# Last mean summed on TensorE, two reciprocals moved from items 1 and 2 to items 5 and 6, x in twelve chunks

## The reference, cut to what matters

```python
x = fft2(x).real                      # x: (2, 3008, 256), over sequence and feature axes
x = x.reshape(6016, 256)
rms = sqrt(mean(x * x, -1) + 1e-6);  xn = x / rms * rms_g
g = xn @ w_gate;  v = xn @ w_val      # 256 -> 1536
x = (g * sigmoid(g) * v) @ w_out      # 1536 -> 256
h = x @ w_in                          # 256 -> 2048
out = (h * cos(h)) @ w_out2           # 2048 -> 256
```

## Time and profile before

| | us |
|---|---|
| median of 3 runs | 985.58 |
| the profiled execution | 985.71 |
| its span in the trace | 983.6 |
| TensorE (PE) busy | 972.8 (99%) |
| VectorE (DVE) busy | 743.0 |
| ScalarE (ACT) busy | 640.0 |
| GpSimd (POOL) busy | 350.5 |

### The profile page before, as it was taken

One profiled execution on the slowest core, in us unless ns is written; L12 is line 12 of the kernel. 1 busy time (PEld: TensorE's weight loads), 2 busy tenths in 40 slices (PEclk: granted clock), 3 DMA queues, 4 the chain that ended last, 5 costly groups with the idle time before them and its releaser, 6 DMA issues.

```text
span 983.6 us, 13016 instructions
## 1 busy us (share of the span) xinstructions
PE 972.8 (99%) x4518; PEld 808.3 (82%) x4518; DVE 743.0 (76%) x1031; ACT 640.0 (65%) x805; POOL 350.5 (36%) x292
## 2 busy tenths in 40 slices
PE   8999999999999999999999999999999999999998
PEld 7987878888888888888888888888888888888886
DVE  6889877768876768877768887667887767887665
ACT  5586778765368774458775448775448776437777
POOL 0378864027730007750007751005661004770000
PEclk9999999999999999999999999999999999999999
DMA  9889001001010001010001010001000000000001
GB/s 326 241 209 246 1 5 50 0 1 43 1 43 1 1 0 42 1 36 6 0 1 42 0 32 11 0 0 42 0 32 0 0 0 3 39 0 0 0 0 42
DMA packets 14082, 36.80 MB, mean 37 GB/s; under 512 B 2618, under 2 KB 6682, under 8 KB 13658
## 3 DMA queue, kind: packets, MB, share of 16 engines
q1 hardware_dynamic: 11978, 31.63, 9.6%
q0 software_dynamic: 2064, 4.72, 2.6%
HBM read 22.35 MB, written 9.26 MB: 32 GB/s over the span
## 4 chain that ended last, share of the span: by engine, by line
PE 95%; DVE 3%; DMA 1%; ACT 1%; SPq 0%; issue 0%; DVEq 0%
PE ps L546 31%; PE ps L548 30%; PE ps L547 30%; PE ps L497 2%; DMA x_sb<-x 1%; PE ps L515 1%; PE ps L513 1%; DVE h_lo L1002 0%; DVE plus L1017 0%; SPq L323 0%; DVE x_sb L907 0%; DVE work L1025 0%; PE ps L482 0%; DVE work L1026 0%; DVE h_lo L1010 0%; PE ps L531 0%
## 5 line engine op out<-in xcount | busy, mean ns | idle before, releaser
L546 PE MATMUL ps<-h_hi,wo_hi 128*128 128x502 f32 x672 | 261.7, 389 | 0.6 <-DVE h_lo L1002 0.5
L548 PE MATMUL ps<-h_hi,wo_lo 128*128 128x502 f32 x672 | 261.6, 389 | 0.0
L547 PE MATMUL ps<-h_lo,wo_hi 128*128 128x502 f32 x672 | 261.0, 388 | 0.0
L1116 POOL TENSOR_TENSOR h_lo<-work,h_hi 128x502 fp32r<-128x502 f32 x92 | 102.7, 1124 | 374.7 <-ACT h_hi L800 373.2
L785 ACT ACTIVATE h_hi<-work 128x502 fp32r<-128x502 f32 x132 | 82.3, 626 | 174.3 <-POOL work L1205 174.2
L1103 DVE SCALAR_TENSOR_TENSOR work<-work,ps 128x1004 f32<-128x1004 f32 (+1 forms) x109 | 117.1, 1075 | 97.5 <-ACT work L885 96.9
L1087 DVE SCALAR_TENSOR_TENSOR work<-work,ps 128x1004 f32<-128x1004 f32 (+1 forms) x109 | 116.5, 1074 | 48.0 <-ACT work L871 48.0
L546 PE MATMUL ps<-x_hi,win_hi 128*128 128x502 f32 x384 | 150.1, 391 | 1.3 <-DVE work L1103 1.3
L547 PE MATMUL ps<-x_lo,win_hi 128*128 128x502 f32 x384 | 149.4, 389 | 0.0
L546 PEld LDWEIGHTS ps<-h_hi,wo_hi 128*128 128x128 f32 x672 | 126.3, 188 | 28.1 <-DVE h_lo L1002 1.1
L548 PE MATMUL ps<-x_hi,win_lo 128*128 128x502 f32 x384 | 149.1, 388 | 0.0
(11 more groups left out here) (90 smaller groups left out, 1279.2 us busy)
## 6 DMA issues: line engine op xcount, KB each, us to landing
out<-y_sb SPq DMA_DIRECT2D x10, 502.0 KB, 3.1
x_sb<-x SPq DMA_DIRECT2D x6, 768.0 KB, 10.9
w_lo<-w_f POOLq DMA_DIRECT2D x6, 512.0 KB, 7.8
uv_t<-uv_dram SPq DMA_DIRECT2D x6, 502.0 KB, 3.7
wo_raw<-wo SPq DMA_DIRECT2D x1, 2048.0 KB, 8.8
win_raw<-win SPq DMA_DIRECT2D x1, 2048.0 KB, 9.1
raw_b<-w1b SPq DMA_DIRECT2D x3, 512.0 KB, 12.6
raw_a<-w1a SPq DMA_DIRECT2D x3, 512.0 KB, 12.9
```

The lines of the kernel that those rows point to most:

```text
L546: nc.tensor.matmul(acc, w_hi, v_hi, start=start, stop=False)
L547: nc.tensor.matmul(acc, w_hi, v_lo, start=False, stop=False)
L548: return nc.tensor.matmul(acc, w_lo, v_hi, start=False, stop=stop)
L1116: nc.gpsimd.tensor_tensor(dst, src, hi.bitcast(F32), ALU.subtract).then_inc(s, 1)
```

## The change

x comes in twelve chunks, and the nine columns m that are folded by half lie elsewhere (chunks 3, 5 and 8 with 3 columns each; before: chunks 3 and 5 with 3 each and chunk 10 with 1). The rows of the second batch's four parts are 5, 4, 4, 4 in place of 4, 4, 4, 5. The ninth mean no longer waits for an addition on GpSimd: TensorE accumulates the product of plane 1 and that of plane 0, and its place is after item 3 in place of item 4 of tile 0. The reciprocals of groups 1 and 2 stand in items 5 and 6 of the second network in place of 1 and 2.

```diff
-CHUNKS = [1, 1, 1, 3, 3, 3, 3, 3, 3, 2, 1]
-HALF_FOLDED = (3, 5, 10)
+CHUNKS = [1, 1, 1, 3, 2, 3, 1, 3, 3, 2, 3, 1]
+HALF_FOLDED = (3, 5, 8)
-PARTS = [[3, 3, 4, 4, 3], [4, 4, 4, 5]]
+PARTS = [[3, 3, 4, 4, 3], [5, 4, 4, 4]]
-        LAST_MEAN_AT = 4
+        LAST_MEAN_AT = 3
@@ rms(q), TensorE
-                pe.wait_ge(sq_added, q + 1)
+                if q < MEANS - 1:
+                    pe.wait_ge(sq_added, q + 1)
+                else:
+                    pe.wait_ge(sq_done, q + 1)
...
-                    nc.tensor.matmul(ps[at:at + QUARTER, rms_bank(q), r * N2:(r + 1) * N2], mean_w,
-                                     squares[:, q % SQUARES, 0, i * N2:(i + 1) * N2], start=True, stop=True
+                    acc, cols = ps[at:at + QUARTER, rms_bank(q), r * N2:(r + 1) * N2], slice(i * N2, (i + 1) * N2)
+                    if q == MEANS - 1:
+                        nc.tensor.matmul(acc, mean_w, squares[:, q % SQUARES, 1, cols], start=True, stop=False)
+                    nc.tensor.matmul(acc, mean_w, squares[:, q % SQUARES, 0, cols], start=q < MEANS - 1, stop=True
                                      ).then_inc(ms_done, 1)
@@ tile(), VectorE, second network
-                    if first and j in (1, 2):
-                        recip(j)
+                    if first and j in (5, 6):
+                        recip(j - 4)
@@ tile(), GpSimd, first network
-                    if first and i == LAST_MEAN_AT - 1:
-                        add_squares(MEANS - 1)
```

## The result

The changed kernel takes 992.2 us (median of 5 runs, 991.4 to 992.49) against 985.58: ratio 1.0066, 95% interval 1.0051 to 1.0081. It is slower by 6.6 us. Its profiled execution takes 992.09 us with a span of 990.0, 6.38 more than that of before.

A forecast was written before the change was run, and what follows sets the result against it. TensorE, busy 972.8 of 983.6 us, was taken as the bound. From 985.71 us, gains of 1.5, 0.2 and 0.1 and a stall of 5.5 gave 989.4; the 8-in-10 range was 987.8 to 992.4.

The forecast's parts named there:

- first rival: TensorE, after the stall: the clock falls to 1.2 GHz, 2.5 us more, 991.9; chance 0.27.
- The stall: TensorE before item 8's up products: late reciprocals delay `scale_uv`, then ScalarE's `split_uv`; 5.5 us lost, bounds 4.6 to 6.5.
- Part 1: Ninth mean, near 83 and 87 us: TensorE's waits for GpSimd's addition and VectorE's low part go; gain 1.5 us.
- Part 2: Chunks and folding: TensorE's folding ends 0.6 us sooner, features start 0.35 sooner; net gain 0.2, bounds -0.4 and 0.6.
- Part 3's small gain: Reciprocals leaving item 1: the slow first matmul there goes, gain 0.1 us.
- VectorE was held up in GpSimd's run: Rival: item 5's low parts are held up in GpSimd's unbroken run, about 1.2 us more, 990.6; chance 0.1.
- `split_uv` did not find its data: Rival claimed the opposite: ScalarE's `split_uv` finds its data, no stall, only the gains count, 983.9 us; chance 0.08.

The follow-up runs named there:

- the spare addition: Kernel with the reciprocals back (983.97 us), plus a GpSimd addition of the old size at the old place, on squares nobody reads: 984.06 us, ratio 0.9988.

## Why the prediction was right in its mechanism and 2.8 us short

The measured 992.2 lies at the upper end of the range and on the first rival (991.9), not on the forecast (989.4).

- **The stall: right.** 5.46 measured for 5.5, `scale_uv` ending at 169.37 for 171.15 - 1.7 of gains = 169.4. One step was wrong without harm: I let the DMA come 1.5 us ahead of GpSimd's queue with the median landing of 3.7. This very load took 5.0 us in the trace of before and 4.8 in that of after, so it came only 0.5 ahead. With 5.0 my sum has it at 161.5 + 1.95 + 5.0 = 168.45, still before 168.7; the stall would have come out the same, by a margin of 0.2.
- **The step that failed: the clock**, which the forecast left out and whose fall it gave a chance of 0.27. My reason against it was that no gap of the trace had lowered the clock; but the longest there was 1.4 us, so the trace had nothing to say on 5:

```profile
133.78 0.39 PE L548 MATMUL ps<-x_hi,win_lo 128*128 128x502 f32 x1
135.43 0.50 PE L546 MATMUL ps<-x_hi,win_hi 128*128 128x502 f32 x1 [1.26 <-DVE work L1103]
```

The changed kernel lost 2.46 us to slow matmuls, and the run with TensorE kept busy takes them away. The rule of the Trainium skill that the rival cites ("TensorE: Matmul & The Clock Gate", section "HAM oscillation — how this bites in real kernels": waiting for data can put the clock back) was borne out. That my size for the rival, 2.5, fits so well is luck: I chose 5 us of slow stretch out of "up to 8", the profile lists a granted clock of 1.00 all through the slow start that it came from the earlier trace rows, so that start is not shown to be the clock's, and behind a gap of the same 5.47 the kernel with only the reciprocals moved lost 1.8.
- **Part 1: right, a little more.** 1.67 (1.73 less the 0.06 that TensorE was ahead at 58 us; 1.68 in the kernel with the reciprocals back) for 1.5. The 16 records of the mean took 77.71 - 77.23 = 0.48 us, not 0.67: 0.030 each, where I had used 0.042. The reason that I gave for VectorE's short operation, that GpSimd has no addition beside it, is not shown: it was as short behind the spare addition.
- **Part 2: the term was mis-sized.** 0.2 forecast, nothing that can be measured. Features started at 26.03, only 0.10 sooner and not 0.35, and both that and the 0.06 at 58 us are far inside what this start varies from one execution to the next:

```profile
24.37 0.44 DVE L933 COPY g_sb<-ps 128x272 f32<-128x272 f32 x1 [0.33 <-PE ps L482]
...
26.03 1.20 PE L497 MATMUL ps<-feat,g_sb 128*96 128x129 f32 x9 [1.01 <-ACT g_sb L681]
```

TensorE's folding did end about 0.5 sooner, so it waited 1.01 for the copies in place of 0.54: the copies on VectorE came only 0.1 sooner (24.37 for 24.47), where my working let the copies take but 0.25 of the 0.6.
- **Part 3's small gain** (0.1 at item 1) came and went: the first of item 3's up products is no longer slow (139.78, 0.39; before 141.50, 0.49), but the first of item 4's comes 0.08 later behind the matmul before it (145.02 to 145.40; before 146.82 to 147.12).
- **The other rivals:** VectorE was held up in GpSimd's run, but little (L1015 took 3.13 for two at 161.61), and not where TensorE needed it. `split_uv` did not find its data.

## What to carry to other kernels

The price of a moved operation is not its own duration but that of the longest chain behind it up to the next in-order queue that something urgent stands in; follow it through every queue, DMA landings included, and compare its end with the slot. Lateness costs little until a queue stops, and two near-equal ways into one operation must both be shortened. A landing time is to be read from the load's own row in its own place, not from the median. Where the bounding engine is TensorE, a gap of some microseconds has to be priced twice, once as idle time and once as slow matmuls after it.

## What the runs showed that was not expected

- A TensorE gap of 2.98 us lowered the granted clock in the traced execution, one of 1.46 did not; behind gaps from 2.98 to 10.54 us the loss by slow matmuls was much the same in the traces, 1.7 to 2.5 us.
- The same load of 502 KB landed 3.7 us after its issue in the median and after 4.8 to 5.0 where two broadcast loads were issued within 0.5 us of it. Moved away from them, to 119.1, it took 3.4 (the run with uv_t's load early).
- A VectorE operation of 0.68 us took 4.75 beside GpSimd once, and 0.68 when a like addition ended just ahead of it.
